# Gated recurrence and squared-ReLU layer on one core: the first product as seven block products (Strassen) instead of eight

## The reference

```python
# x: [2, 6080, 256], f_logit alike, lower_bound: [256]
f = lower_bound + (1 - lower_bound) * sigmoid(f_logit)
for t in range(6080):                      # per batch and channel
    h = f[:, t] * h + (1 - f[:, t]) * x[:, t]
    y[:, t] = h
z = y.reshape(12160, 256) @ w_in           # [256, 2048]
g = relu(z) ** 2
out = g @ w_out                            # [2048, 256]
```

## Time and profile before

| | |
|---|---|
| times of three executions | 1077.82 us median (1077.4, 1077.82, 1078.49) |
| span of the profiled execution, first to last instruction | 1077.1 us (0.7 us under the median) |
| mean granted TensorE clock in it | 0.997 |
| PE busy, matmuls | 1068.6 us, 99% of the span, 4622 instructions |
| DVE busy | 591.0 us, 55% |
| ACT busy | 525.1 us, 49% |
| POOL busy | 1.4 us |
| HBM traffic | 41.6 MB, 39 GB/s over the span |

### The profile page before, as it was taken

The page is one execution under the profiler, slowest core; times in us unless marked ns, Lnnn a source line. Parts: engine busy times, 40 slices in busy tenths (PEclk is TensorE's granted clock), DMA queues, the critical chain, the costliest instruction groups (busy, mean ns, idle before and its releaser), DMA issues.

```text
span 1077.1 us, 13223 instructions
## 1 busy us (share of the span) xinstructions
PE 1068.6 (99%) x4622; PEld 871.5 (81%) x4622; DVE 591.0 (55%) x1067; ACT 525.1 (49%) x873; POOL 1.4 (0%) x6
## 2 busy tenths in 40 slices
PE   8999999999999999999999999999999999999998
PEld 5998888888888888888888888888888888888887
DVE  6765554655546555465554655646556455565533
ACT  5555454454444445445454454544544445444443
POOL 0000000000000000000000000000000000000000
PEclk8999999999999999999999999999999999999999
DMA  7110101101001011010110101101011010100000
GB/s 264 40 57 1 57 22 37 59 0 58 28 31 58 0 58 40 19 58 0 58 50 9 58 13 46 58 0 58 19 39 58 0 58 19 39 19 0 21 19 20
DMA packets 21343, 41.75 MB, mean 39 GB/s; under 512 B 1360, under 2 KB 3152, under 8 KB 21328
## 3 DMA queue, kind: packets, MB, share of 16 engines
q1 hardware_dynamic: 21296, 41.56, 11.0%
q0 software_dynamic: 32, 0.00, 0.0%
HBM read 29.10 MB, written 12.45 MB: 39 GB/s over the span
## 4 chain that ended last, share of the span: by engine, by line
PE 98%; DVE 1%; DMA 0%; ACT 0%; issue 0%; POOL 0%; POOLq 0%
PE out_ps L435 49%; PE hidden_ps L419 49%; DMA bound<-lower_bound_t 0%; PE hidden_ps L402 0%; DVE y L316 0%; DVE neg_input L306 0%; DVE forget L298 0%; DVE g_lo L360 0%; DVE y_hi L326 0%; ACT square L271 0%; ACT result L247 0%; ACT relu L266 0%; POOL zeros L385 0%; DVE g_hi L358 0%; DVE state L325 0%
## 5 line engine op out<-in xcount | busy, mean ns | idle before, releaser
L266 ACT ACTIVATE relu<-hidden_ps 128x512 f32<-128x512 f32 (+1 forms) x384 | 227.8, 593 | 524.1 <-PE hidden_ps L419 519.8
L358 DVE CAST g_hi<-square 128x512 fp32r<-128x512 f32 (+1 forms) x384 | 162.9, 424 | 460.5 <-ACT square L271 460.4
L435 PE MATMUL out_ps<-g_hi,w_out_hi 128*128 128x512 f32 (+1 forms) x768 | 301.3, 392 | 0.8 <-DVE g_lo L360 0.8
L435 PE MATMUL out_ps<-g_hi,w_out_lo 128*128 128x512 f32 (+1 forms) x768 | 301.1, 392 | 0.0
L435 PE MATMUL out_ps<-g_lo,w_out_hi 128*128 128x512 f32 (+1 forms) x768 | 301.1, 392 | 0.0
L419 PE MATMUL hidden_ps<-y_lo,w_in_hi 128*128 128x512 f32 (+1 forms) x762 | 299.0, 392 | 0.0
L419 PE MATMUL hidden_ps<-y_hi,w_in_lo 128*128 128x512 f32 (+1 forms) x762 | 299.0, 392 | 0.0
L419 PE MATMUL hidden_ps<-y_hi,w_in_hi 128*128 128x512 f32 (+1 forms) x762 | 299.0, 392 | 0.0
L360 DVE TENSOR_TENSOR g_lo<-square,g_hi 128x512 fp32r<-128x512 f32 (+1 forms) x384 | 263.9, 687 | 13.2
L271 ACT ACTIVATE square<-relu 128x512 f32<-128x512 f32 (+1 forms) x384 | 240.9, 627 | 14.2 <-DVE g_lo L360 0.5
L435 PEld LDWEIGHTS out_ps<-g_hi,w_out_hi 128*128 128x128 f32 x768 | 144.7, 188 | 33.2 <-issue 1.2
(11 more groups left out here) (24 smaller groups left out, 68.0 us busy)
## 6 DMA issues: line engine op xcount, KB each, us to landing
f_in<-f_logit_t SPq DMA_DIRECT2D x22, 512.0 KB, 4.1
x_in<-x_t SPq DMA_DIRECT2D x22, 512.0 KB, 4.8
out_t<-result SPq DMA_DIRECT2D x21, 512.0 KB, 3.1
w_in_raw<-w_in_t SPq DMA_DIRECT2D x2, 512.0 KB, 7.9
w_out_raw<-w_out_t SPq DMA_DIRECT2D x2, 512.0 KB, 8.7
out_t<-result SPq DMA_DIRECT2D x2, 448.0 KB, 2.9
w_in_raw<-w_in_t SPq DMA_DIRECT2D x1, 640.0 KB, 10.4
w_out_raw<-w_out_t SPq DMA_DIRECT2D x1, 640.0 KB, 11.4
```

The lines of the kernel that those rows point to most:

```text
L266: nc.scalar.activation(relu[:, k, 0:n], hidden_ps[:, s % HBANKS, 0:n], ACT.Relu).then_inc(relu_done, 1)
L358: nc.vector.tensor_copy(g_hi[:, slot, 0:n], square[:, k, 0:n]).then_inc(g_hi_done, 1)
L435: mm = nc.tensor.matmul(out_ps[:, b, c, 0:n], w[:, j, c * P:(c + 1) * P], v[:, r % GSLOTS, 0:n], start=(j == 0 and w is w_out_hi and v is ...
```

## The change

Two batches' tiles (the columns) and two halves of the hidden units (M = 2) form a 2x2 block product with the two channel chunks as the inner dimension: z11, z21 are the two hidden halves of batch 0, z12, z22 those of batch 1. The seven-product scheme makes four blocks of z from seven block products instead of eight.

- **Quads.** The unit of work is now a "quad": one block of 128 hidden units of each half, for both batches, which is the work of four steps before. A tile has QUADS = 8 quads j = 0 to 7; 12 tiles give 96 quads, 8 of them with 448 columns, 88 with 512. PE has 7 x 3 matmuls of the first product in a quad (24 in four steps before) and 8 x 3 of the second, as before.
- **One bank, read in between.** P1 opens a bank (two take turns), ACT copies it out to `p1`; the next product adds to the same bank and gives u2 = P1 + ..., copied out to `u2`; the next u3, copied to `u3`; the fourth makes z21, which ACT takes out with ReLU. P2, P5 and P3 are in other banks; DVE adds them to `p1`, `u3`, `u2` and gets z11, z22, z12 (P5 and P3 are chained in one bank too). PE waits for each copy before it adds to the bank. Between these products it does the second product of the quad before.
- **Operands.** Four sums of y blocks (t1 to t4) per tile on DVE, with their hi and lo parts (seven operands, in two sets by tile parity); four sums of w_in blocks on POOL, in four pieces (CUTS in quads: 1, 1, 2, 4), with hi parts on ACT and lo parts on DVE.
- **Wider instructions.** ReLU, square, g_hi and g_lo of a batch's pair of blocks are single instructions of 1024 columns, but for batch 0's ReLUs. g_hi of batch 1 is made on ACT.
- **In place.** The gate, the recurrence and the sums t overwrite `f_in` and `x_in`, so a tile's loads wait for the sums' parts of the tile before.
- WARM_UP is 18; `first_steps` is gone.

The diff, cut to its core ("+" lines; they take the place of the functions of the same engine shown above):

```diff
+CUTS = (0, 1, 2, 4, 8)
+WARM_UP = 18
+A11, A12, A22, S2, S3, S4, S1 = range(7)
+B11, B21, B22, T1, T2, T3, T4 = range(7)
+BANK_P2, BANK_P5 = 2, 3
...
+        @block.sync
+            def load(it):
+                sp.wait_ge(y_ready, 5 * (it - 1) + 3)
+                sp.wait_ge(t_done, 4 * it)
+                sp.wait_ge(state_done, 4 * it)
+                for b in range(B):
+                    load_x(it, b)
+                sp.wait_ge(y_ready, 5 * it)
+                for b in range(B):
+                    load_f(it, b)
...
+            load_first(0, 0)
+            load_w_in(0)
+            load_first(0, 1)
+            load_first(1, 0)
+            load_first(1, 1)
+            load_w_out(0)
+            for q in range(1, len(CUTS) - 1):
+                load_w_in(q)
+                load_w_out(q)
+            load(1)
...
+        @block.scalar
+            def plain_w_in_hi(q):
+                act.wait_ge(w_in_loaded[q], 32)
+                nc.scalar.copy(wc_hi[:, A11:A12 + 1, piece(q)], w_in_raw[:, :, 0, piece(q)]
+                               ).then_inc(w_plain_hi_done, 1)
+                nc.scalar.copy(wc_hi[:, A22, piece(q)], w_in_raw[:, 1, 1, piece(q)]).then_inc(w_plain_hi_done, 1)
+            def sum_w_in_hi(q):
+                act.wait_ge(w_sum_done, 4 * (q + 1))
+                for c in range(C):
+                    nc.scalar.copy(wc_hi[:, S2 + 2 * c:S2 + 2 * c + 2, piece(q)], w_in_raw[:, c, :, piece(q)]
+                                   ).then_inc(w_sum_hi_done, 1)
...
+            def copy_out(it, b):
+                if not narrow(it):
+                    act.wait_ge(stored[b], 16 * it)
+                for c in range(C):
+                    if c == 0:
+                        act.wait_ge(out_done[b], it + 1)
+                    else:
+                        act.wait_ge(g_used[b], QUADS * (it + 1))
+                    nc.scalar.copy(result[:, b, c, 0:n], out_ps[:, b, c, 0:n]).then_inc(result_done[b], 1)
+            def quad(it, odd, j):
+                act.wait_ge(p1_done, q + 1)
+                nc.scalar.copy(p1[:, 0:n], hidden_ps[:, a, 0:n]).then_inc(p1_copied, 1)
+                if not first:
+                    relu_pair1(*before(it, j))       # waits for c22_added, c12_added of that quad
+                    square_pair1(*before(it, j))
+                act.wait_ge(u2_done, q + 1)
+                nc.scalar.copy(u2[:, 0:n], hidden_ps[:, a, 0:n]).then_inc(u2_copied, 1)
+                if not first:
+                    hi_pair1(*before(it, j))
+                act.wait_ge(u3_done, q + 1)
+                nc.scalar.copy(u3[:, 0:n], hidden_ps[:, a, 0:n]).then_inc(u3_copied, 1)
+                act.wait_ge(c11_added, q + 1)
+                nc.scalar.activation(h[0][:, 0, 0:n], h[0][:, 0, 0:n], ACT.Relu).then_inc(relu_done[0], 1)
+                act.wait_ge(c21_done, q + 1)
+                nc.scalar.activation(h[0][:, 1, 0:n], hidden_ps[:, a, 0:n], ACT.Relu).then_inc(c21_copied, 1)
+                nc.scalar.square(h[0][:, :, 0:n], h[0][:, :, 0:n]).then_inc(square_done[0], 1)
+                if narrow(it):
+                    if j == 0:
+                        plain_w_in_hi(1)
+                        sum_w_in_hi(1)
+                        round_w_out(1)
+                    if j == 1:                        # pieces 2 likewise
...
+                    if j == 2:
+                        plain_w_in_hi(3)
+                        sum_w_in_hi(3)
+                    if j == 3:
+                        round_w_out(3)
+                else:
+                    if j == 0:
+                        copy_out(it - 1, 0)
+                    if j == 1:
+                        copy_out(it - 1, 1)
+                if not last(it) and j < B * C:
+                    gate(it + 1, j // C, j % C)
...
+        @block.vector
+            def quad(it, odd, j):
+                dve.wait_ge(p1_copied, q + 1)
+                dve.wait_ge(p2_done, q + 1)
+                nc.vector.tensor_tensor(h[0][:, 0, 0:n], hidden_ps[:, BANK_P2, 0:n], p1[:, 0:n], ALU.add
+                                        ).then_inc(c11_added, 1)
+                if not last(it):
+                    ahead(it + 1, 1 - odd, j)         # forget, neg_input, state, y parts and sums
+                if not first:
+                    lo_pair(*before(it, j), 1)        # waits for hi_pair1
+                dve.wait_ge(u3_copied, q + 1)
+                nc.vector.tensor_tensor(h[1][:, 1, 0:n], hidden_ps[:, BANK_P5, 0:n], u3[:, 0:n], ALU.add
+                                        ).then_inc(c22_added, 1)
+                if not last(it):
+                    ahead_late(it + 1, 1 - odd, j)    # the scan in j = 1 to 4
+                dve.wait_ge(p3_done, q + 1)
+                nc.vector.tensor_tensor(h[1][:, 0, 0:n], hidden_ps[:, BANK_P5, 0:n], u2[:, 0:n], ALU.add
+                                        ).then_inc(c12_added, 1)
+                hi_pair0(it, j)                       # waits for square_done[0]
+                lo_pair(it, j, 0)
+                if narrow(it):
+                    if j == 0:
+                        plain_w_in_lo(1)
+                        sum_w_in_lo(1)
+                        rest_of_w_out(1)
...
+            for b in range(B):
+                for c in range(C):
+                    forget_part(0, b, c)
+                    input_part(0, b, c)
+                    scan_part(0, b, c)
+                    state_part(0, b, c)
+                    if b == 0:
+                        plain_part(0, 0, c)
+                    if (b, c) == (0, 0):
+                        plain_w_in_lo(0)
+            t1(0)
+            t2(0)
+            sum_w_in_lo(0)
+            plain_part(0, 0, 2)
+            sums_hi_part(0, 0, 0)
+            sums_lo_part(0, 0, 0)
+            t3(0)
+            t4(0)
+            sums_hi_part(0, 0, 1)
+            sums_lo_part(0, 0, 1)
+            rest_of_w_out(0)
...
+        @block.gpsimd
+            def w_in_sums(q):                         # four tensor_tensor, each waits for the one before
+                pool.wait_ge(w_plain_ready, 2 * q + 2)
...
+        @block.tensor
+            def second(it, j, b, m, c):
+                if m == 0 and c == 0:
+                    if narrow(it) and j in CUTS and b == 0:
+                        pe.wait_ge(w_out_ready, CUTS.index(j) + 1)
+                    if j == 0 and not narrow(it):
+                        pe.wait_ge(result_done[b], C * it)
+                    pe.wait_ge(g_ready[b], q + 1)
...
+            def quad(it, odd, j):
+                prev = None if first else before(it, j)
+                wait_y(it, j, 1)
+                wait_w(it, j, w_plain_ready, 2)
+                if not (narrow(it) and j < 2):
+                    pe.wait_ge(c21_copied, q - 1)
+                product(it, odd, j, a, A11, B11, True, p1_done)
+                wait_y(it, j, 2)
+                if not first:
+                    pe.wait_ge(c11_added, q)
+                product(it, odd, j, BANK_P2, A12, B21, True, p2_done)
+                if not first:
+                    second(*prev, 0, 0, 0)
+                wait_y(it, j, 4)
+                wait_w(it, j, w_sum_ready, 2)
+                pe.wait_ge(p1_copied, q + 1)
+                product(it, odd, j, a, S2, T2, False, u2_done)
+                if not first:
+                    pe.wait_ge(c12_added, q)
+                product(it, odd, j, BANK_P5, S1, T1, True, p5_done)
+                if not first:
+                    second(*prev, 0, 0, 1)
+                wait_y(it, j, 5)
+                pe.wait_ge(u2_copied, q + 1)
+                product(it, odd, j, a, S3, T3, False, u3_done)
+                if not first:
+                    second(*prev, 0, 1, 0)
+                    second(*prev, 0, 1, 1)
+                pe.wait_ge(u3_copied, q + 1)
+                product(it, odd, j, a, A22, T4, False, c21_done)
+                if not first:
+                    second(*prev, 1, 0, 0)
+                pe.wait_ge(c22_added, q + 1)
+                product(it, odd, j, BANK_P5, S4, B22, False, p3_done)
+                if not first:
+                    second(*prev, 1, 0, 1)
+                    second(*prev, 1, 1, 0)
+                    second(*prev, 1, 1, 1)
```

More of the change, by code:

```diff
@@ L136, in run @@
[L136 to L154, removed]
@@ new lines, in program, with run @@
+        result_done = [sem(f"result_done{b}") for b in range(B)]
+        block = ctx.enter_context(nc.Block())
+        def run(eng, quad):
+            for s in range(2 * QUADS):
+                quad(s // QUADS, s // QUADS, s % QUADS)
+            with eng.Fori(1, IT // 2 - 1) as k:
+                for s in range(2 * QUADS):
+                    quad(k * 2 + s // QUADS, s // QUADS, s % QUADS)
+            for s in range(2 * QUADS):
+                quad(IT - 2 + s // QUADS, s // QUADS, s % QUADS)
@@ L290, in _ @@
+            gate(0, 0, 0)
+            gate(0, 0, 1)
+            plain_w_in_hi(0)
+            gate(0, 1, 0)
```

(33 more changed lines are left out.)

548 lines of the change are left out of this document (305 added, 243 removed).

## The result

The changed kernel takes 1084.1 us (median of 4, 1082.3 to 1087.5) against 1078.2 beside it (median of 4): ratio 1.006, 95% interval 1.0042 to 1.0078. It is slower, as forecast, and within the range, but by 0.6% where I had said 2.2%. The profiled execution took 1083.8, its span is 1082.0 us at a mean clock of 0.974.

A forecast was written before the change was run, and what follows sets the result against it. The prediction took PE, busy 99% of the span, to bound the kernel. It summed 1077.1 - 66.3 + 41 + 33.4 + 4.4 + 11 = 1100.6, plus 0.7 to the median: 1101 us, range 1076 to 1130.

The forecast's parts named there:

- Matmuls removed, -66.3: PE's quads: 45 matmuls instead of 48, at 0.2325 us wide and 0.204 narrow, save 66.3 us if PE stays the bound.
- u2, +4.4: ACT's copy of u2 releases PE slightly late for U3: 0.05 us a quad over 88 quads, +4.4 us.
- the walk: Estimated queue times, in quads and opening; in a quad, u2's copy done at 3.98, PE released 4.20, U3 due 4.19.
- The stall, +33.4: Quad j = 1: PE's second product waits 3.04 us for ACT's late batch 1 result copy, in eleven tiles: +33.4 us.
- The clock, +11: Behind each tile's stall the granted clock may fall: 1.0 us a tile, +11 us, bounds 0 and 37.
- the rival that took its warning for every tile: Rival B: clock falls at every stall, low as long as in the opening: +26 on top, 1127 us; chance 0.15.
- The opening and the end, +41: First quads wait on weight and sum queues, +40.3; last second products wait 1.0 for g_lo: +41 us, bounds 25 and 55.
- DVE and ACT keep up: In the quads, DVE at some 80% and ACT at some 75% busy still fit, but for u2.
- Rival D: Opening costs 20 us less than forecast and no stall drops the clock: 1070 us, faster; chance 0.12.
- B: Rival: clock falls at every stall and stays low as long as in the opening: +26 us, 1127; chance 0.15.
- C: Rival: ACT becomes the bound at u2, wide ReLU or square 0.15 us longer: +22 us, 1123; chance 0.10.

The follow-up runs named there:

- early_relu_first: Changed kernel with batch 1's result copy directly behind the copy of u3, and pair 1's ReLU ahead of ACT's copy of P1: 1044.15 us.
- before_small_last: The kernel before with its four small tensors (bound, slope, middle, state) allocated last in SBUF: 1055.2 us, ratio 0.979.
- after_weights_later: The changed kernel with its weights allocated behind x_in, f_in and the small tiles, as the kernel before has them: 1094.6 us.
- combined: Changed kernel with batch 1's copy behind u3, small tensors last, unchanged w_in parts one quad ahead, pair 1's ReLU before P1's copy: 1015.5 us, ratio 0.941.
- copy_mid: Changed kernel with batch 1's result copy between ACT's two ReLUs and its square of pair 0 in quad j = 1: 1065.2 us, ratio 0.989.
- stagger: Changed kernel with hi and lo parts of the unchanged w_in blocks made one quad earlier than the sums: 1074.5 us, ratio 0.996.

## Why the prediction was right in sign and too high

- **Matmuls removed, -66.3 at 0.2325 and 0.204 each.** The number was right (4338 instructions in the page). The step "the distance is 0.2325, so a wide quad is 10.46 us" failed: I carried a row of the kernel before over to a kernel with another layout of SBUF. With u2 in time (early_relu_first) a quad of this layout takes 10.328 us where 45 x 0.2325 is 10.463: 88 x 0.135 = **11.9 us**, the largest part of the miss, and it has nothing to do with seven products. Nobody who reads only the earlier trace rows can see it; the two kernels allocate their tensors in another order, which the prediction leaves out, and the distance should have had a range. That the layout sets it is shown on both kernels (before_small_last, after_weights_later); why it does stays open.
- **u2, +4.4.** A quad without a stall takes 10.372 us in the changed kernel, against those 10.328: **3.9** over 88. The mechanism was right: released at 4.20 in the walk, due at 4.19. In the trace the copy of u2 ends at 3.99 where the walk has 3.98, and the waits of the weight load (15.4 us in 81) bear the late release out.
- **The stall, +33.4.** (13.41 - 10.37) x 11 = 33.4. Place, length and number as forecast.
- **The clock, +11, bounds 0 and 37.** Four falls x 1.6 = **6.4**. I had a loss of 1.0 in every tile; it was 1.6 in four of eleven. A fall lasts half as long as in the earlier trace rows: the granted clock is low from 313.3 to 316.7 us in the tile shown, 3.4 us, against 6.8 in the opening of the kernel before. There the first products came with pauses, here PE had no gap behind the stall; that this is the reason was not tested. The Trainium skill (TensorE: Matmul & The Clock Gate, Loop structure matters more than you think) has as its bad case a long wait between every matmul and the next; here PE waits once a tile, and the rival that took its warning for every tile did not come true: four of eleven lost the clock.
- **The opening and the end, +41.** What is left of the measured difference: 1082.0 - 1077.1 + 66.3 + 11.9 - 3.9 - 33.4 - 6.4 = **39.4**. The starts of the first wide matmul say the same: 120.5 us less 336 matmuls of 0.204 is 51.9, and 88.5 less 366 of them is 13.9 in the kernel before, 38 apart. For POOL's four sums of 512 columns the walk had 4.8 us (twice 1.03 ns a column, and 0.15 us each); the trace has 5.3, and one of them takes 1.8 times DVE's 693 ns. The Trainium skill (GPSIMD Engine Reference, Engine selection) gives about twice for two inputs, and this trace agrees.
- **DVE and ACT keep up.** 67% and 66% busy, not the 75 to 80 I gave at the end: I counted their fullest quads for all. No wait of PE's for them in a wide quad but u2 and the copy.
- Rival D, a cheaper opening, did not come; B and C neither. The 11.9 us came from a cause that was no rival of mine.

The misses, 11.9 + 4.6 (clock) + 0.5 (u2) + 1.6 (opening), are the 18.6. They look large because 78 us of gain (66.3 and 11.9) and 83 of cost nearly cancel: the net of such terms is no better known than its worst one.

What did the scheme itself do, then? With equal offsets in both, the kernel before takes 1055.2 us and the changed one, with stall and late u2 mended and a part of the opening, 1015.5: 3.8% less. In the wide tiles the gain is larger, 10.88 to 10.20 us for the work of a quad, 60 us over 88, which is the three matmuls in 48; some 25 us of it still go to the opening, which combined leaves longer than that of the kernel before. As written, the change gave it all back, 40 at one misplaced copy and 39 in the opening.

## What to carry to other kernels

When a copy frees a buffer for the next tile, find the consumer's slot in the other engine's order and put the copy before it in its own queue: here two lines moved up by one product were worth 40 us. Put small tensors behind the large ones in SBUF, and check the offset of the moving operands against the weights: here that was worth 22 us in a kernel that the profile showed as 99% busy. And when single edits are priced, look at the quad in the trace, not only at the time: a wait can be worth nothing alone and 10 us once PE is faster.

## What the runs showed of the hardware

- The distance between float32r matmuls of 512 columns, each with its own weight load, was 0.2267, 0.2289 or 0.2324 us with moving operands 0 or 512, 64, 128 bytes off the weights, the tensors of ScalarE and VectorE moving with them. PE reads as 99% busy in all of them.
- The granted clock fell behind 16 of 33 stalls in which PE was idle for 2.8 us (4, 5 and 7 of eleven in the traces of three kernels) and behind none of eleven of 1.65 us (copy_mid). Where it fell the quad took 1.6 us longer, and three times 2.8 (twice in stagger, once in after_weights_later). In the tile shown the low stretch is 3.4 us and begins 1.3 us after PE has started again.
- VectorE's tensor_tensor took 692 ns with one input in PSUM and 693 with both in SBUF; GpSimd's took 1261 ns for the same 512 columns.
